# Keys' head rows made on TensorE instead of loaded, and carried matmuls on four tiles, in a recurrent attention and mixture-of-experts kernel

## The reference

```python
state = np.zeros((B, H, D, D), dtype=np.float32)
for t in range(S):
    kt, vt, rt = (k[:, :, t], v[:, :, t], r[:, :, t])
    cur = np.einsum('bhd,bhe->bhde', u[None] * kt, vt)
    y[:, :, t] = np.einsum('bhd,bhde->bhe', rt, state + cur)
    state = w[None, :, :, None] * state + np.einsum('bhd,bhe->bhde', kt, vt)
...
logits = x @ phi
...
slot_input = d.T @ x
...
    h = np.maximum(slot_input[e] @ w1[e], 0.0)
    slot_out[e] = h @ w2[e]
...
r = np.maximum(h, 0.0)
g = r * r
return (g @ w_out).astype(np.float32)
```

## Time and profile before

| what | value |
|---|---|
| time of three runs | 424.39 us median (421.39 to 436.14) |
| the profiled execution | 427.77 us, its span 425.7 us |
| TensorE busy | 378.1 us (89%) |
| VectorE, ScalarE, GpSimd busy | 262.5, 182.0, 58.0 us |
| moved by DMA | 55.43 MB, mean 130 GB/s |
| mean granted clock | 0.968 of full speed |

### The profile page before, as it was taken

The page is one execution under the profiler, slowest core; times in us unless marked ns, Lnnn a source line. Parts: engine busy times, 40 slices in busy tenths (PEclk is TensorE's granted clock), DMA queues, the critical chain, the costliest instruction groups (busy, mean ns, idle before and its releaser), DMA issues.

```text
span 425.7 us, 11855 instructions
## 1 busy us (share of the span) xinstructions
PE 378.1 (89%) x4840; PEld 334.1 (78%) x4840; DVE 262.5 (62%) x420; ACT 182.0 (43%) x312; POOL 58.0 (14%) x83
## 2 busy tenths in 40 slices
PE   0387889977889889878999999999999999999997
PEld 0277688775878333437999999999999999999996
DVE  7375568887876371149765756665565666566653
ACT  3012335242434210264555554645464555556552
POOL 3222132433321011038000000000000000000000
PEclk9998999998999899985999999999999999999999
DMA  6998799999992999970000200100020001002002
GB/s 154 261 249 240 216 260 266 256 254 246 257 235 86 355 372 375 406 269 0 2 1 2 74 2 0 53 22 0 0 74 0 0 31 42 0 0 74 0 2 74
DMA packets 28599, 55.43 MB, mean 130 GB/s; under 512 B 3360, under 2 KB 22816, under 8 KB 28192
## 3 DMA queue, kind: packets, MB, share of 16 engines
q1 hardware_dynamic: 28576, 55.11, 44.7%
HBM read 50.38 MB, written 4.72 MB: 129 GB/s over the span
## 4 chain that ended last, share of the span: by engine, by line
PE 76%; issue 11%; DMA 4%; SPq 2%; POOL 2%; DVE 2%; ACT 1%; DVEq 0%; POOLq 0%; ACTq 0%
PE out_ps L1120 49%; PE h_ps L1098 5%; PE score_ps L844 4%; PE y_ps L864 4%; DMA w_w<-in_w 3%; PE y_ps L882 3%; PE inc_ps L855 2%; PE x_ps L833 2%; DMA rk<-in_rk_t 2%; POOL state_a L406 2%; PE wide L1036 1%; PE wide L988 1%; SPq L344 1%; PE lg_ps L819 1%; PE lg_ps L826 1%
## 5 line engine op out<-in xcount | busy, mean ns | idle before, releaser
L1120 PE MATMUL out_ps<-w_hi,act_hi 128*128 128x384 f32 x384 | 131.2, 342 | 3.5 <-DVE act_lo L801 1.7
L1120 PE MATMUL out_ps<-w_hi,act_lo 128*128 128x384 f32 x384 | 131.6, 343 | 0.0
L1120 PE MATMUL out_ps<-w_lo,act_hi 128*128 128x384 f32 x384 | 131.4, 342 | 0.0
L796 DVE TENSOR_TENSOR act<-relu_h 128x512 f32<-128x512 f32 x96 | 68.8, 717 | 78.0 <-ACT relu_h L569 78.0
L569 ACT ACTIVATE relu_h<-h_ps 128x512 f32<-128x512 f32 x96 | 57.4, 598 | 101.1 <-PE h_ps L1098 101.1
L1120 PEld LDWEIGHTS out_ps<-w_hi,act_hi 128*128 128x128 f32 x384 | 73.2, 191 | 4.9 <-issue 2.9
L1120 PEld LDWEIGHTS out_ps<-w_lo,act_hi 128*128 128x128 f32 x384 | 73.4, 191 | 3.8
L1120 PEld LDWEIGHTS out_ps<-w_hi,act_lo 128*128 128x128 f32 x384 | 73.1, 190 | 0.0
L801 DVE TENSOR_TENSOR act_lo<-act,act_hi 128x512 fp32r<-128x512 f32 x96 | 68.4, 712 | 4.9 <-ACT act_hi L572 1.0
L572 ACT ACTIVATE act_hi<-relu_h 128x512 fp32r<-128x512 f32 x96 | 60.9, 634 | 3.9
L460 ACT ACTIVATE x_t<-y_ps 112x512 f32<-112x512 f32 x24 | 14.3, 598 | 77.1 <-PE y_ps L882 77.1
(11 more groups left out here) (145 smaller groups left out, 391.7 us busy)
## 6 DMA issues: line engine op xcount, KB each, us to landing
w_sb<-in_w SPq DMA_DIRECT2D x21, 512.0 KB, 7.8
rk<-in_rk_t SPq DMA_DIRECT2D x48, 192.0 KB, 7.8
w_room<-in_w SPq DMA_DIRECT2D x4, 1536.0 KB, 12.9
keys_in<-in_rkv_n SPq DMA_DIRECT2D x24, 192.0 KB, 7.9
values<-in_rkv_n SPq DMA_DIRECT2D x24, 192.0 KB, 7.1
out_dram<-y_sb SPq DMA_DIRECT2D x5, 768.0 KB, 3.5
w_x<-in_w SPq DMA_DIRECT2D x2, 1536.0 KB, 13.6
w_w<-in_w SPq DMA_DIRECT2D x4, 768.0 KB, 12.0
```

The costliest lines, as they stand in the source:

```text
L796: nc.vector.tensor_tensor(act[f % 2][:, :], relu_h[f % 2][:, :], relu_h[f % 2][:, :], ALU.mult).then_inc(act_done, 1)
L1120: last = nc.tensor.matmul(out_ps[t][:, 0:DM], a[f % 4][:, tok], w[:, f], start=(f == 0 and i == 0), stop=(f == NF - 1 and i == 2))
```

## The change

1. rk goes. Receptances alone are loaded with head rows (recept, six buffers, two transfers of 96 KB). The keys with head rows are made on the chip: keys_n, now four buffers with each head on 64 columns, is transposed by TensorE into the bank kt_ps (L870 in the new file, four transposes per unit, two units ahead of its scores), and ScalarE scales it into keys (keep_keys). VectorE's scaling of keys (L642) goes.
2. keys_in has two buffers for three. SP issues keys_in(n+2) and recept(n+2) behind values(n), and keys_in(n+2) waits until GpSimd has turned keys_in(n).
3. Odd batches write head h to column group 1 - h of y_ps. Carried is issued in two halves of 8 matmuls, one before and one behind the state step, the second with a wait for the first (carried_half). Own, the x copy (two instructions for one) and the router's first product (8 matmuls of 256 columns for 4 of 512) follow the swap; phi is loaded in both head orders.
4. kt_ps takes the bank of the logits, which now share x_ps with the turned x. GpSimd's copy of the state moves from behind keys_n(n+2) to behind keys_n(n+4).
5. The loop covers chunks 1 to 4; chunk 5 is written out behind it (it leaves out the key transposes of its last two pairs). Behind it the router's product comes before the turn of the last x.

```diff
-RK_BUFS = 3
-K_BUFS = 3
+R_BUFS = 6
+K_BUFS = 2
...
-    rk = [place(f"rk{i}", [P, 2, B, P]) for i in range(RK_BUFS)]
+    recept = [place(f"recept{i}", [P, B, P]) for i in range(R_BUFS)]
     w2_at = cursor[0]
     keys = [place(f"keys{i}", [P, B, P]) for i in range(2)]
-    keys_n = [place(f"keys_n{i}", [P, B, 2 * D]) for i in range(2)]
+    keys_n = [place(f"keys_n{i}", [P, B, 2, SECOND]) for i in range(HP)]
...
+            def load_keys(n):
+                c, hp = n // HP, n % HP
+                wait(sp, kn_done, n - K_BUFS + 1)
+                sp.dma_start(keys_in[n % K_BUFS][:, :, :], rkv_n[c, hp][:, 1]).then_inc(keys_in_in[n % K_BUFS], 16)
+            def load_receptances(n):
+                c, hp = n // HP, n % HP
+                wait(sp, q_done, n - R_BUFS + 1)
                 for half, rows in enumerate(HEAD_ROWS):
-                    sp.dma_start(phi_sb[rows, :, :], phi.rearrange("(a h d) s -> h d a s", h=2, d=D)[half]).then_inc(params_in, 16)
+                    sp.dma_start(recept[n % R_BUFS][rows], rk_t[c, hp, half][:, 0]).then_inc(recept_in[n % R_BUFS], 16)
+            sp.wait_ge(cleared, 1)
+            load_keys(0)
+            load_receptances(0)
+            load_params()
+            load_keys(1)
+            load_receptances(1)
...
                 sp.dma_start(values[n % V_BUFS][:, :, :], rkv_n[c, hp][:, 2]).then_inc(values_in[n % V_BUFS], 16)
+                if n + 2 < UNITS:
+                    load_keys(n + 2)
+                    load_receptances(n + 2)
...
-                wait(pool, inc_done, n - 1)
-                nc.gpsimd.tensor_tensor(keys_n[n % 2][:, :, :], keys_in[n % K_BUFS][:, :, :],
-                                        kn_pow[:, hp].rearrange("p h d -> p (h d)").unsqueeze(1).broadcast_to([P, B, 2 * D]),
+                wait(pool, inc_done, n - HP + 1)
+                nc.gpsimd.tensor_tensor(keys_n[n % HP][:, :, :, 0:D],
+                                        keys_in[n % K_BUFS][:, :, :].rearrange("p b (h d) -> p b h d", h=2),
+                                        kn_pow[:, hp].unsqueeze(1).broadcast_to([P, B, 2, D]),
...
-                if 2 <= n < UNITS - HP + 2:
-                    keep_state(n - 2)
+                if 4 <= n < UNITS - HP + 4:
+                    keep_state(n - 4)
...
+            def keep_keys(n):
+                sc.wait_ge(kt_mm, n + 1)
+                wait(sc, score_done, n - 1)
+                nc.scalar.activation(keys[n % 2][0:PAIR], kt_ps[0:PAIR, :].rearrange("p (b t) -> p b t", t=P), ACT.Copy,
+                                     scale=w_64_inv[0:PAIR, n % HP:n % HP + 1]).then_inc(k_done, 1)
...
+            for tile in recept:
+                nc.vector.memset(tile[SUB // 2:SUB], 0.0)
+            for tile in keys_n:
+                last = nc.vector.memset(tile[:, :, :, D:], 0.0)
+            last.then_inc(cleared, 1)
...
-                ve.wait_ge(rk_in[n % RK_BUFS], 32 * (n // RK_BUFS + 1))
-                wait(ve, score_done, n - 1)
-                nc.vector.tensor_tensor(
-                    keys[n % 2][0:PAIR].rearrange("p b (s t) -> p (b s) t", t=SUB),
-                    rk[n % RK_BUFS][0:PAIR, 1].rearrange("p b (s t) -> p (b s) t", t=SUB),
-                    k_pow[0:PAIR, hp].unsqueeze(1).broadcast_to([PAIR, 2 * B, SUB]), ALU.mult).then_inc(k_done, 1)
+                ve.wait_ge(recept_in[n % R_BUFS], 32 * (n // R_BUFS + 1))
                 wait(ve, carried_done, n - Q_BUFS + 1)
                 nc.vector.tensor_tensor(
                     queries[n % Q_BUFS][0:PAIR].rearrange("p b s k t -> p (b s) k t")[:, :, 0],
...
+            def turn_keys(i):
+                for b in range(B):
+                    last = nc.tensor.transpose(kt_ps[:, P * b:P * (b + 1)],
+                                               keys_n[i][:, b].rearrange("p h d -> p (h d)"), ident[:, :])
+                last.then_inc(kt_mm, 1)
...
+            def head_rows(b, h):
+                return HEAD_ROWS[h ^ (b % 2)]
+            def carried(hp, b, h, s):
+                state = state_b if s else state_a
+                at = BANK * s + SUB * b
+                return nc.tensor.matmul(y_ps[head_rows(b, h), at:at + SUB], state[HEAD_ROWS[h], hp, b],
+                                        queries[hp][HEAD_ROWS[h], b, s, 0], start=(s == b % 2 and b < 2), stop=False,
+                                        skip_group_check=True)
...
+                    s = (b + half) % 2
+                    if s or not first:
+                        for h in range(2):
+                            last = carried(hp, b, h, s)
+                last.then_inc(carried_done if half else carried_half, 1)
...
-            with pe.Fori(1, CH) as c:
+            def chunk(c, last_chunk):
                 for hp in range(HP):
                     n = c * HP + hp
+                    carried_step(n - 1, (hp - 1) % HP, False)
                     state_step(n, hp, c)
-                    carried_step(n - 1, (hp - 1) % HP, False)
+                    carried_rest(n - 1, (hp - 1) % HP, False)
                     if hp == 1:
-                        pe.wait_ge(lg_free, c)
-                        pair_logits()
+                        pe.wait_ge(x_done, n - 2)
+                        pair_logits(x_ps)
+                    if hp == 2:
+                        pe.wait_ge(lt_done, c)
+                        pe.wait_ge(x_done, n - 2)
+                        token_logits(x_ps)
                     scores_step(n, hp)
                     own_step(n - 1, (hp - 1) % HP, False)
-                    turn_step(n - 2, (hp - 2) % HP)
+                    if hp == 1:
+                        pe.wait_ge(lt_done, c)
                     if hp == 2:
-                        pe.wait_ge(lt_done, c)
-                        token_logits()
+                        pe.wait_ge(lg_free, c + 1)
+                    turn_step(n - 2, (hp - 2) % HP, x_ps)
+                    if hp < 2 or not last_chunk:
+                        keys_step(n + 2, (hp + 2) % HP)
+            with pe.Fori(1, CH - 1) as c:
+                chunk(c, False)
+            chunk(CH - 1, True)
             carried_step(UNITS - 1, HP - 1, False)
+            carried_rest(UNITS - 1, HP - 1, False)
             own_step(UNITS - 1, HP - 1, False)
-            turn_step(UNITS - 2, HP - 2)
+            turn_step(UNITS - 2, HP - 2, x_ps)
+            pe.wait_ge(y_copied, UNITS)
+            pe.wait_ge(k_done, UNITS)
+            pair_logits(kt_ps)
+            turn_step(UNITS - 1, HP - 1, y_ps)
```

More of the change, by code:

```diff
@@ L228, in program @@
         state_a_ready = sem("state_a_ready")
+        carried_half = sem("carried_half")
         carried_done = sem("carried_done")
@@ L854, in unit_state @@
                             at = BANK * s + D * b
[L855 removed]
+                            last = nc.tensor.matmul(inc_ps[rows, at:at + D], keys_n[hp][part, b, h, 0:D],
                                                     values[hp][part, b, D * h:D * (h + 1)], start=True, stop=True)
                 last.then_inc(inc_done, 1)
[L859 to L876 removed]
```

161 lines of the change are left out of this document (81 added, 80 removed).

## The result

The changed kernel took 429.42 us (median of 4 runs, 427.09 to 430.91) beside 423.88 us of the kernel before (median of 4, 421.39 to 436.14); the ratio is 1.015, with a 95% interval of 1.007 to 1.022. Both intervals lie within 2% of no change but for the upper edge of the first, and the two don't agree on whether there is a small loss. The forecast was 428 us, range 419 to 438, no change that shows. The time came out near the forecast; several terms of the sum did not, and they cancelled.

What follows compares the result with a forecast made beforehand. Bound by new-code pauses, then data waits, up to the last own step: 40.5 + 24.0 + 51.0 + 23.6 = 139.1 us against 137.1, +2.0. On 427.8 profiled or 424.4 median: 429.8 or 426.4, so 428, range 419 to 438.

Steps and rivals of the forecast that it cites:

- What bounds the kernel: Head stage: new code pauses first, later loop runs wait for data; the end moves one for one with last own step.
- TensorE's unit: Each unit of the loop: key transposes add 0.51 us, carried on four tiles saves 0.24, net +0.27 us.
- Rival D: Carried step: four tiles bring nothing, as weight loads hold its matmuls; a unit is 4.05 us, total 433.8; chance 0.10.
- DMA: Loop runs 2 to 4: 1.11 MB a unit at 257 to 266 GB/s, so 17.0 us each, a gain of 5.5.
- Start: Chunk 0: late values of unit 1 cost +2 us, transposes +1, so it ends at 40.5 for 37.5.
- E: Start costs 5 us and the last chunk's pauses bring the lower clock; 433.5 us, chance 0.08.
- C: Pauses of all new code halve, none in the last chunk, start costs nothing; 416 us, chance 0.10.
- Last chunk: Copied chunk behind the loop: 18.2 us plus five new-code pauses of 1.18, less 0.5, makes 23.6 us.
- rival B: Copied last chunk doesn't pause, 5.4 us less than the sum; 422.6 us, chance 0.15.
- F: Loop body, 24 matmul records longer, no longer stays in and pauses each run; 444 us, chance 0.05.
- The number: Whole kernel: 428 us, no change that shows, halfway between 429.8 and 426.4; chance 0.52.

Runs made afterwards that it cites:

- e7: Changed kernel with heads not swapped for odd batches, so carried and own matmuls use two tiles; 436.09 us against 427.84 of the kernel before, ratio 1.019.
- e9: Changed kernel with last chunk in the loop, three key buffers and each w1 load three units later; 419.76 us for 430.23 of the kernel before.
- e2: Changed kernel with its last chunk back in the loop, two key transposes of old data extra; 424.18 us, the changed kernel 426.67.
- e4: Kernel before with only its last chunk written out behind the loop; 431.54 us for 428.24, ratio 1.013.
- e6: Kernel before without loading the keys with head rows from unit 3 on; 414.25 us for 427.84, ratio 0.966.

## Why the prediction was right, and which of its steps were not

The forecast of each stage, and what it was (us; the two traces of each kernel):

| stage | forecast | changed | before |
|---|---|---|---|
| end of chunk 0 | 40.5 | 44.4, 45.0 | 37.5, 37.2 |
| first run of the loop | 24.0 | 23.4, 24.0 | 23.2, 25.4 |
| runs 2 to 4 | 51.0 | 47.7, 47.7 | 56.5, 57.1 |
| last chunk | 23.6 | 20.5, 20.2 | 19.9, 21.5 |
| last own step ends | 139.1 | 136.0, 136.9 | 137.1, 141.2 |

- **What bounds the kernel: right.** Waits for data in the loop, pauses of new code ahead of it, and an end that follows the last own step: over the fourteen traces that step ends at 123.4 to 141.9 us, and what follows takes 288.6 to 291.6. That is one for one within 3 us; the five traces in which it ends before 133.5 all have 290.9 or more behind it, so a us or two of such a gain may be lost there.
- **TensorE's unit: the mechanism right, the sum 0.28 us too high.** Keys cost 0.53 (0.51 said), carried saved 0.26 (0.24 said). Left out: the own step goes on four tiles too (0.74 to 0.59), the x step is shorter with other transposes behind it (0.53 to 0.44), the scores take 0.89 for 0.98 and the state 0.50 for 0.45. The net of +0.27 came out as -0.01. Rival D, no gain from four tiles, is refuted by e7.
- **DMA: the floor of 16.8 to 17.3 us for four units was wrong.** The step took the rate of a loop that waits for data, 257 to 266 GB/s, as the most there is. The changed loop moved 289 GB/s in its third run, 4.63 MB in 16.0 us at a DMA share of 0.92, and TensorE didn't wait. The 17.0 us said for a run stood on this floor and on the unit's sum alike; both were too high, and runs 2 to 4 took 47.7 us for 51.0.
- **Start: the term was +3 and measured 6.9 to 7.8.** The late values were right (the bytes from the release on are 1.11 MB, not 1.09, which changes little), and unit 1 began at 24.9, a little behind the 22 to 24 given. I then added 1 us for transposes, of which those ahead of unit 2 took 0.90 to 1.12 us each in place of 0.53, and nothing for longer pauses or for TensorE's clock: 20.75 us busy where e9 needs 14.32 for the same matmuls. No rival had a start that runs slow. E put 5 us on the start without a mechanism, and the lower clock on the last chunk, where the granted clock was 1.00. C, with half the pauses and no cost of the start, falls: the pauses of the start and the first run were 8.55 us for 7.06. This was the largest error, and it hid what the loop gained beyond the forecast.
- **Last chunk: pauses yes, size no.** 23.6 was said, 20.2 to 20.5 measured. The pauses are there (2.0 and 1.6 us on issue in the two traces), and e2 shows the copy to cost 2.8 to 3.1 us of the stage, so rival B falls. They were priced at five of 1.18, those of a stretch where transfers compete, and here the DMA share is 0.30. (Four fetches stand in the stretch.) e4 shows that the price was not absurd: in the kernel before, with the transfers still running, the same copy cost 3.3 to 4.9. The Trainium skill ("Runtime: NRT & Kernel Launch", "Instruction fetch mechanics") calls the crossing of a block mostly hidden and prefers unrolling to a branch; on TensorE here the copy was dearer than the branch in both kernels, by 2.8 to 4.9 us.
- **F (the loop body no longer stays in)** falls: no instruction packet on queue 8 in 67.8 to 115.5 us.

- **The number: in part luck.** Against the sum, chunk 0 ended 3.9 to 4.5 us late, runs 2 to 4 took 3.3 less and the last chunk 3.1 to 3.4 less. The errors nearly cancel; without that of the start the last own step would have been forecast some 6 to 7 us too late.

So, counted from the trace of e6, whose last own step ends at 123.4: +9.2 for a start that runs late and slow, +0.9 in the first run, +0.2 for TensorE's added work in three runs, +2.3 in the last chunk, which makes 136.0.

## What to carry to other kernels

Before judging such a trade, price the relief alone by leaving the transfer out: here that showed 13.6 us, of which the change kept almost nothing, and sent the search from the loop to the start. A buffer count that makes the issuing engine stand in the first units costs more than the wait seen there, so count the transfers that queue behind it. Keep a repeated chunk in the loop, where its code is already in: this and one more buffer gave back 7 to 8 of the 12.6 us. Let work that has to be added fall under a wait that is there anyway.

## What the hardware showed that I had not expected

- TensorE's rate in the first 25 us of the head stage: 14.3 to 21.1 us busy for the same 445 to 448 matmul records, with a mean granted clock of 1.00 and 0.87. Behind long pauses on issue stand stretches at the lower level (0.54 from 32.5 to 36.1 us). Steps at half rate stand also where the granted clock reads 1.00 (unit 1 of the changed kernel and of the kernel before).
- Fetches of code show as packets on a queue of their own, some four to five for 20 to 25 us of new code. The pauses that go with them vary from 0.5 to 4.5 us between traces of like kernels. The longest stands where the transfers of data keep the DMA engines full (4.54 us at a share of 1.07, in e4), but a light load doesn't always make them short: e9 has one of 2.34 us, from 45.67 on, at a share of 0.01.
- VectorE's busy time for the same 24 or 25 instructions of a run of the loop was 13.7 to 16.9 us in the runs that wait for data, and 13.3 to 13.5 in e6, where 192 KB a unit were no longer loaded. The cause is open: GpSimd's busy time is longer in the same stretches too (6.8 to 7.9 us for 5.3, with the same eight instructions).
